# Attention work of TensorE placed between the first and the second GEMM's step of a slot

## The reference

```python
mag = np.sqrt(a_re * a_re + a_im * a_im)
scale = np.minimum(mag, 0.999) / (mag + 1e-06)
...
for t in range(S):
    new_re = ar * S_re - ai * S_im
    new_im = ar * S_im + ai * S_re
    S_re, S_im = (new_re + kv, new_im)          # kv = k_t (outer) v_t
    y[:, :, t] = np.einsum('bhd,bhde->bhe', q[:, :, t], S_re)
...
h = x @ w_in                                     # 384 -> 2048
g = h * np.clip(h + 3.0, 0.0, 6.0) / 6.0
x = g @ w_out                                    # 2048 -> 384
...
h = (x @ w1) * (x @ w2) @ w3                     # 384 -> 1024 -> 1024
return (h @ w_out2)                              # 1024 -> 384
```

## Time and profile before

| | us |
|---|---|
| runs (median of 3) | 1011.91 (1009.15 to 1012.15) |
| the profiled execution | 1009.13 |
| its span, first to last instruction | 1007.3 |
| PE busy in the span | 960.0 (95%) |
| DVE, ACT, POOL busy | 528.4, 422.3, 364.9 |
| units 0 to 7 start at | 110.19, 188.68, 264.65, 341.10, 417.07, 493.52, 569.51, 643.91 |
| the second MLP starts at | 699.70 |

### The profile page before, as it was taken

How to read it: one execution, slowest core, us unless ns; L and a number is a source line. 1 busy time by engine, 2 the same in 40 slices (tenths; PEclk the granted TensorE clock), 3 DMA queues, 4 the chain that set the end, 5 groups by cost and what they waited for, 6 DMA issues and landing times.

```text
span 1007.3 us, 15116 instructions
## 1 busy us (share of the span) xinstructions
PE 960.0 (95%) x5913; PEld 877.4 (87%) x5913; DVE 528.4 (52%) x669; ACT 422.3 (42%) x674; POOL 364.9 (36%) x296
## 2 busy tenths in 40 slices
PE   6887699999999999999999999999999999999997
PEld 3556699999999999999999999999888888888886
DVE  5669869669669669669669654242212121212110
ACT  4364554554555554554554533363222121212121
POOL 0353543543543552543553533253222222222221
PEclk9999799999999999999999999999999999999999
DMA  9254411311311221221221020421001010101000
GB/s 352 69 167 117 149 40 41 104 46 40 98 53 40 84 68 40 79 71 41 71 80 40 24 79 25 160 99 42 15 1 63 1 63 1 63 1 63 1 32 33
DMA packets 55913, 66.84 MB, mean 66 GB/s; under 512 B 4896, under 2 KB 50208, under 8 KB 55840
## 3 DMA queue, kind: packets, MB, share of 16 engines
q1 hardware_dynamic: 55840, 65.84, 20.5%
HBM read 45.37 MB, written 11.01 MB: 56 GB/s over the span
## 4 chain that ended last, share of the span: by engine, by line
PE 80%; issue 7%; DVE 5%; ACT 3%; POOL 3%; DMA 1%; SPq 1%; ACTq 0%; POOLq 0%; DVEq 0%
PE acc L737 15%; PE hb L717 14%; PE hb L916 10%; PE acc L938 8%; PE bR L916 5%; PE bQ L916 5%; PE bR L830 3%; POOL gL L1310 3%; PE bP L938 2%; PE bR L801 2%; PE acc L864 2%; PE bQ L801 2%; PE bQ L823 2%; PE bQ L820 2%; PE bQ L784 1%
## 5 line engine op out<-in xcount | busy, mean ns | idle before, releaser
L1310 POOL TENSOR_TENSOR gL<-g_sb,gH 128x384 fp32r<-128x384 f32 x128 | 155.4, 1214 | 253.5 <-ACT gH L1016 209.5
L717 PE MATMUL hb<-xHL,winH 128*128 128x384 f32 x768 | 162.8, 347 | 3.9 <-DMA xHL<-yHL 3.9
L1358 POOL TENSOR_TENSOR pL<-p_sb,pH 128x512 fp32r<-128x512 f32 x48 | 67.0, 1395 | 232.0 <-ACT pH L1098 232.0
L717 PEld LDWEIGHTS hb<-xHL,winH 128*128 128x128 f32 x768 | 133.6, 191 | 5.0 <-DMA xHL<-yHL 4.6
L1230 DVE SCALAR_TENSOR_TENSOR g_sb<-t_sb,hb 128x384 f32<-128x384 f32 x128 | 70.2, 549 | 123.7 <-ACT t_sb L1034 72.1
L737 PE MATMUL acc<-gH,woutH 128*128 128x384 f32 x384 | 129.1, 336 | 4.1 <-ACT gH L1016 2.6
L737 PE MATMUL acc<-gH,woutL 128*128 128x384 f32 x384 | 128.6, 335 | 0.0
L737 PE MATMUL acc<-gL,woutH 128*128 128x384 f32 x384 | 128.3, 334 | 0.0
L1034 ACT ACTIVATE t_sb<-hb,cst 128x384 f32<-128x384 f32 x128 | 74.5, 582 | 89.7 <-PE hb L717 89.5
L1016 ACT CAST gH<-g_sb 128x384 fp32r<-128x384 f32 x128 | 65.4, 511 | 86.5 <-DVE g_sb L1230 85.7
L717 PE MATMUL hb<-xHL,winL 128*128 128x384 f32 x384 | 87.7, 336 | 0.0
(11 more groups left out here) (163 smaller groups left out, 2000.2 us busy)
## 6 DMA issues: line engine op xcount, KB each, us to landing
xHL<-yHL SPq DMA_DIRECT2D x48, 144.0 KB, 2.6
AR<-in_a_re_dram SPq DMA_DIRECT2D x8, 576.0 KB, 3.9
AI<-in_a_im_dram SPq DMA_DIRECT2D x8, 576.0 KB, 5.1
q_sb<-in_q_dram SPq DMA_DIRECT2D x24, 192.0 KB, 2.5
k_sb<-in_k_dram SPq DMA_DIRECT2D x24, 192.0 KB, 3.1
v_sb<-in_v_dram SPq DMA_DIRECT2D x24, 192.0 KB, 2.4
x_dram<-x_sb SPq DMA_DIRECT2D x24, 192.0 KB, 2.7
out_dram<-o_sb SPq DMA_DIRECT2D x6, 768.0 KB, 4.3
```

Of the source, the lines that this page charges most:

```text
L717: mm = pe.matmul(o, w[:, kk * DF1 + ft * P:kk * DF1 + (ft + 1) * P], xv(u)[:, 2 * kk + part, :], start=(i == 0), stop=(i == 8))
L1310: pool.tensor_tensor(gL[:, (n % 3) * UNIT:(n % 3 + 1) * UNIT], g_sb[:, :], gH[:, (n % 3) * UNIT:(n % 3 + 1) * UNIT].bitcast(F32), ALU.subt ...
L1358: pool.tensor_tensor(pL[:, (n % 3) * UNIT2:(n % 3 + 1) * UNIT2], p_sb[:, (n % 2) * UNIT2:(n % 2 + 1) * UNIT2], pH[:, (n % 3) * UNIT2:(n % ...
```

## The change

In the main loop of PE's block, `gemm2(n - 2)` is called behind the attention work of the slot and not ahead of it. A slot was `gemm1`, `gemm2`, attention; it is now `gemm1`, attention, `gemm2`. Slots without attention work and slots 0 and 1 of unit 0, which have no `gemm2`, stay as they are. No other engine's list is changed, and no wait is added or taken away: each moves with its block.

```diff
                     if n is not None:
                         gemm1(u, n)
 
-                    if n is not None and n >= 2:
-                        gemm2(n - 2)
                     if (g := chunk(u, sl, "YU")) is not None:
                         Y(g, 0)
                         Y(g, 1)
...
                         halves_sums(p)
                     if p < NU and sl in angle_slots(p):
                         angle_sums(p, angle_slots(p).index(sl))
+                    if n is not None and n >= 2:
+                        gemm2(n - 2)
                     if u < 0:
                         for m in w3_products(u, sl):
                             w3_product(m)
```

## The result

| | before | after |
|---|---|---|
| runs, median (lowest to highest), us | 1011.72 (1009.15 to 1012.15) | 1020.12 (1019.23 to 1020.94) |
| ratio, with its 95% interval | | 1.0088 (1.0069 to 1.0108) |
| span of the profiled execution, us | 1007.3 | 1019.2 |

A forecast was written before the change was run, and what follows sets the result against it. PE was taken as the bound, busy 960.0 of 1007.3 us, so only its waits could change. The terms 4.0 + 1.56 - 0.6 gave +4.9 us, 1016.8 us on the median 1011.91, range 1011.0 to 1021.5.

The forecast's parts named there:

- signs that I had named for being wrong: Slot 0's sines starting too early, Qb taking 0.95 us there, or new PE idle at TK or in slots 6 to 12.
- Part 1: Slot 2 of units 1 to 6: TQ would wait for Qb, losing 0.66 us a unit, +4.0 us in six.
- Part 2: Slot 2 of unit 0: TQ still starts at 121.19, and `gemm2` becomes work after the wait, +1.56 us.
- rival (d): Unit 0: PE's slow-clock stretch grows by the whole `gemm2`, +1.6 us more, 1018.4 us; chance 0.08.
- Part 3: Start of unit 7: the first `gemm1`'s 0.61 us wait for y in xHL goes, -0.6 us.
- Part 4: Everything else, at nothing: slots 6 and 10 keep their cover, slot 12's wait stays at 0.3 to 0.5 us.
- rival (c): Slots 9 to 12: DVE becomes the bound, slot 12 adds up to 0.90 us a unit; total +10.3, 1022.2; chance 0.11.
- The sum: Whole kernel: 4.0 + 1.56 - 0.6 = +4.9 us, giving 1016.8 us on the runs' median of 1011.91.
- (a): Slot 2: Qb is early, a unit gains 0.59 us; whole kernel -2.6 us, 1009.3; chance 0.12.
- (b): Slot 2: Qb does not move, a unit loses 1.23 us; whole kernel +8.3 us, 1020.2; chance 0.14.
- (e): Whole kernel: PE is full, the covers hold everywhere and nothing shows, 1011.9 us; chance 0.05.

The follow-up runs named there:

- e6: The kernel before, with the second GEMM's step moved behind the attention work in slots 13 and 15 alone; 1006.64 us, ratio 0.9958.

## Why the end of L1158 did not move

DVE's chain in the changed kernel runs about 0.6 us ahead of before from slot 0 to slot 10, and behind L1151 the lead is gone, because L1151 takes 0.6 us longer. I took POOL's L1310 beside it as the cause, and cut that one instruction down; the kernel then leaves out the low part of one step in 16 for 352 of 384 tokens. (L1310 is L1312 here; DVE's and PE's lines keep their numbers.)

```diff
+                w = 32 if n % FT1 == 10 else UNIT
+                o = (n % 3) * UNIT
-                pool.tensor_tensor(gL[:, (n % 3) * UNIT:(n % 3 + 1) * UNIT], g_sb[:, :],
-                                   gH[:, (n % 3) * UNIT:(n % 3 + 1) * UNIT].bitcast(F32),
+                pool.tensor_tensor(gL[:, o:o + w], g_sb[:, 0:w], gH[:, o:o + w].bitcast(F32),
                                    ALU.subtract).then_inc(s["hswish_low"], 1)
```

> The changed kernel, with GpSimd's L1310 in slot 10 of each unit cut from 384 to 32 columns: the low part of the hidden layer's step 10 is left out for 352 of 384 tokens. Theory (VectorE's L1151 takes 2.04 us in the changed kernel because it overlaps this L1310 by 0.8 us): L1151 takes 1.44, L1158 ends 0.6 us earlier (61.05 in even units), the wait at the angle sums falls from 1.02 to about 0.4 us in units 0 to 5 and the total by 3.6 us to 1016.5. Rival (L1151 is long for another reason): its 2.04 us and the 1020.1 us stay.

Measured: 1016.42 us (1015.77 to 1018.18), ratio 1.0059 (1.0044 to 1.0073); 3.7 us less than the changed kernel. DVE and PE in unit 4:

```profile
477.41 0.25 POOL L1312 TENSOR_TENSOR gL<-g_sb,gH 128x32 fp32r<-128x32 f32 x1 [7.77 <-ACT gH L1016]
...
477.60 1.36 DVE L1151 SCALAR_TENSOR_TENSOR W<-W,W 128x1152 f32<-128x1152 f32 x1
...
480.73 2.04 DVE L1158 TENSOR_TENSOR TL<-W,TH 128x1152 fp32r<-128x1152 f32 x1
...
482.86 0.41 PE L852 MATMUL bP<-TH,cstR 128*128 128x384 f32 x1 [0.34 <-issue]
```

L1151 takes 1.36 us, L1158 ends 60.98 us after the unit's start, and the wait at the angle sums is 0.34 instead of 1.02. DVE did gain on the way; where its instruction came to lie beside POOL's, the gain was lost. The Trainium skill (GPSIMD Engine Reference, Specifications) names SBUF interfaces shared by the two engines, and this run agrees: L1151 takes 2.04 us beside the whole L1310 and 1.36 beside the short one. Units 1 to 5 are still 0.73 to 0.88 us longer than before: as much as slot 2 is.

## A version faster than both

The useful part of the change is in slots 13 and 15. There the U and the angle sums come early, which brings forward what slots 0 to 2 wait for, and no wait of PE has its cushion taken away. The edit is made on the kernel before; its lines against the changed kernel:

```diff
+            G2_LAST = (13, 15)
...
+                    if n is not None and n >= 2 and sl not in G2_LAST:
+                        gemm2(n - 2)
...
+                    if n is not None and n >= 2 and sl in G2_LAST:
+                        gemm2(n - 2)
```

> The kernel before, with the second GEMM's step behind the attention work in slots 13 and 15 alone. Theory (slots 13 and 15 are what lets Qb and the emptying of the acc banks come 0.58 us earlier in slots 0 to 2, and nothing is taken from TQ's cushion): the 0.43 us wait in slot 2 of units 1 to 6 goes, slot 2 is 4.03 us instead of 4.58, VectorE moves with PE so that L1158 ends at 61.1 and slot 12 keeps its 0.31 us, unit 7's wait of 0.61 goes: 1010.7 - 3.3 - 0.7 = 1006.7. Rival (L1158 stays at 61.65): slot 12 gives the gain back, 1010.0.

Measured: 1006.64 us (1004.64 to 1008.05), ratio 0.9958 (0.9945 to 0.9971). Slot 2 is 4.0 us, L1158 ends at 61.04 (unit 4), the wait in slot 12 is 0.31, unit 7 starts without a wait: every term as expected. Units 1 to 6 are 4.3 us shorter in all. The profiled execution, the lowest of the five, has something more: in unit 0, PE waits for Qb in slot 2 as before (2.34 us; 2.36 in the kernel before), but its clock is 1.00 behind the wait where it was 0.50, and slots 2 and 3 take 10.67 us instead of 11.93. That is not the new order, which leaves these two slots as they were.

With slots 8 and 9 moved as well (`G2_LAST = (8, 9, 13, 15)`):

> As e6, and the second GEMM's step is also behind the attention work in slots 8 and 9, so that VectorE's unbroken work of slots 8 to 12 can start 0.7 us earlier. Theory (L1151 then runs beside GpSimd's L1310 of slot 10 and takes 2.04 us instead of 1.44, as in the changed kernel): L1158 comes at best 0.1 us earlier, the wait at the angle sums stays near 0.3 us, the total is e6's within 1 us. Rival (VectorE is not slowed by GpSimd): L1158 comes 0.7 us earlier, the wait of slot 12 vanishes, 2.1 to 2.5 us less than e6.

Measured: 1005.04 us (1003.54 to 1006.39), ratio 0.9941 (0.9930 to 0.9953), 1.6 us under the last one by the medians, and 0.24 to 0.30 us less in each of units 1 to 5; neither theory has it. DVE and POOL in slots 10 to 12 of unit 4:

```profile
470.41 1.36 DVE L1154 SCALAR_TENSOR_TENSOR W<-W,W 128x1152 f32<-128x1152 f32 x1 [0.17 <-ACT W L986]
472.74 0.56 DVE L1233 SCALAR_TENSOR_TENSOR g_sb<-t_sb,hb 128x384 f32<-128x384 f32 x1 [0.97 <-POOL gL L1313]
...
470.86 1.78 POOL L1313 TENSOR_TENSOR gL<-g_sb,gH 128x384 fp32r<-128x384 f32 x1 [8.56 <-PE acc L737]
```

L1151 (here L1154) started 1.2 us earlier and stayed short. This time POOL's instruction was the long one, 1.78 us instead of 1.0, and `hswish` of the next slot stood 0.97 us for it. L1158 came only 0.25 us earlier, enough to end the wait in slot 12. I had named the overlap rightly and the engine that pays for it wrongly.

## Why the prediction was right, and where it was not

The direction was right, and 1020.1 us lies in the range, near its upper end; the forecast of +4.9 us was little more than half of the measured +8.4. One of the signs that I had named for being wrong did come: new idle time between slots 6 and 12, at the angle sums.

- **Part 1, TQ in slot 2.** The local working held. The chain is bound by slot 0's L1034, it gained 0.58 us (0.57 forecast), PE stood 1.17 us for Qb, and the slot became 0.8 us longer (0.66). The sum counted this as six units' loss. Whether it is one hangs on slot 12. With the old order there, a unit is only 0.2 to 0.4 us longer than before, because the lag is given back where PE used to stand. With the new order and L1310 cut down it comes out whole, 0.73 to 0.88 us in each of units 1 to 5. In unit 6, which has no angle sums, the gain at the unit's end covers it.
- **Part 2, TQ of unit 0.** Forecast 1.56, measured 1.56 over slots 2 and 3 (11.93 to 13.49); PE stood 3.93 us. Its clock was down behind the wait in both kernels, and for no more time in the changed one, so the clock did not add to it, and rival (d) falls. Unit 0's slot 12 adds 0.61. The other 0.4 us of the unit lie mostly in slot 0, which differed from kernel to kernel (3.72 to 4.41) whatever stood in slots 2 to 12.
- **Part 3, unit 7.** Its wait of 0.61 is gone. Unit 6 with its end is 0.07 shorter, as +0.8 in slot 2 and -0.8 in slot 15 cancel.
- **Part 4, "everything else, at nothing".** This step failed, and in one place. I let DVE's chain in slots 9 to 12 shift with the scores and kept the wait of slot 12 at 0.3 to 0.5. It was 1.02. PE came early and L1158 did not. That is what rival (c) foresaw, to which I gave 0.11, at up to 0.90 us a unit, though not by its reason: DVE's work did shift, by 0.6 us, and the part was right on that up to L1151. It missed that L1151 would then run beside POOL's L1310, although I had weighed just such an overlap for Qb.
- **The sum.** What was missing in it is the overlap that Part 4 put at nothing, and the run with L1310 cut down prices it: without the overlap the kernel is 3.7 us faster than the changed one and 5.3 us slower than the runs of before beside it, near the forecast +4.9 (6.4 by the lengths from unit 0's start, where unit 0 has 2.1 instead of 1.56). The same can be read from the end of L1158. A unit that still waits at the angle sums grows by 1.56 us if `gemm2` stands behind them, less what L1158 ends earlier. For unit 4: changed kernel 1.56 - 0.01 = 1.55, measured 1.55; L1310 cut down 1.56 - 0.67 = 0.89, measured 0.86; slot 2 alone 0 + 1.24, measured 1.24; slots 13 and 15 alone 0 - 0.61, measured 0.61 shorter. The forecast had L1158 gain 0.9 us and got 0.66 a unit; it gained nothing in the even units and 0.15 in the odd ones, and units 1 to 5 grew by 1.42 to 1.57.
- **Rivals (a), (b), (e)** fall: Qb moved by 0.58, neither 1.56 nor 0. That (b)'s +8.3 us is close to the measured 8.4 is chance; its mechanism is not in the trace.

Left open: what makes the stretch before unit 0 differ by up to 2.5 us between executions. That it does shows in the starts; why was not tried. Open too is why the same wait in unit 0 brought the clock down in some executions and not in others.

## What to carry to other kernels

A block of work that never waits is worth most directly ahead of the wait that ends last in a period. Moving it behind that wait can cost its whole length, however small the wait was: here 1.56 us, for a wait of 0.31. What comes back is only what the awaited instruction then ends earlier, so measure its end from the period's start in both kernels. When an engine gains a lead, look at what its instructions come to lie beside: a lead of 0.6 us was lost in one instruction here. Move such a block only in the slots whose results are wanted early, one by one, rather than in all of them by one rule.

## What the runs showed of the hardware

- A VectorE and a GpSimd instruction with SBUF inputs that overlap by 0.8 to 0.9 us cost one of them 0.6 to 0.8 us: L1151 2.04 us instead of 1.36 to 1.44 beside L1310, or L1310 1.78 instead of 1.0 beside L1151. In both runs the one that started second was the one that got longer: DVE's, 0.19 us behind POOL's, and POOL's, 0.45 us behind DVE's.
- PE's clock fell to half after 1.63 us of standing in the three odd units of one kernel (the stretch's mean is 0.57), and did not in the even units, after the same idle time. The half clock cost 1.6 us each time. In slot 2 of unit 0 it fell after 2.23 to 2.36 us in three kernels and stayed up after 2.34 to 2.41 us in three others, all with the old order there; after 1.73 us in slot 2 of units 1 and 3 to 6 of another kernel it stayed up as well. So the length of the idle time alone did not decide it.
